# Turning batch 0's tokens with VectorE's 32x32 blocks and DMAs instead of TensorE

## What is computed

```python
y = h * sigmoid(conv(h)) @ w_out                       # h = relu(x @ w_in); 2 x 768 x 512
xn = (y - mean) / sqrt(var + 1e-6) * g_ln              # over the 512 features
out = y + relu(xn @ w_ch1) @ w_ch2                     # 512 -> 2048 -> 512
```

## Time and profile before

| | us |
|---|---|
| median of 3 runs | 467.7 |
| lowest, highest | 467.66, 473.04 |
| the profiled execution | 469.79 |
| its span | 468.1 |

### The profile page before, as it was taken

One profiled execution on the slowest core, in us unless ns is written; L12 is line 12 of the kernel. 1 busy time (PEld: TensorE's weight loads), 2 busy tenths in 40 slices (PEclk: granted clock), 3 DMA queues, 4 the chain that ended last, 5 costly groups with the idle time before them and its releaser, 6 DMA issues.

```text
span 468.1 us, 8636 instructions
## 1 busy us (share of the span) xinstructions
PE 454.7 (97%) x3119; PEld 401.5 (86%) x3119; DVE 279.7 (60%) x631; ACT 199.3 (43%) x499; POOL 269.5 (58%) x409
## 2 busy tenths in 40 slices
PE   7899889999999999999999999999999999999997
PEld 6677668999898988989889889989998999899985
DVE  4879875787676887894675543466662334243333
ACT  2988978534325756435432154224310331233110
POOL 3645788999975000077988886870024588878100
PEclk9999999999999999999999999999999999999999
DMA  9988772121201100001124432220020202220003
GB/s 226 185 200 180 185 194 60 46 86 50 91 0 46 46 1 0 1 0 45 47 91 124 124 64 95 90 81 11 1 112 22 83 10 91 90 86 6 1 0 134
DMA packets 74501, 35.17 MB, mean 75 GB/s; under 512 B 57408, under 2 KB 68700, under 8 KB 74460
## 3 DMA queue, kind: packets, MB, share of 16 engines
q1 hardware_dynamic: 70588, 33.66, 26.2%
q10 hardware_dynamic: 3872, 0.97, 0.9%
HBM read 28.72 MB, written 3.15 MB: 68 GB/s over the span
## 4 chain that ended last, share of the span: by engine, by line
PE 85%; DVE 5%; SPq 3%; issue 3%; ACT 1%; ACTq 1%; DMA 1%; POOL 0%; DVEq 0%; POOLq 0%
PE two L1493 9%; PE two L1494 9%; PE two L1492 9%; PE two L1469 8%; PE two L1472 8%; PE two L1471 8%; PE two L1319 5%; PE two L1321 5%; PE two L1320 5%; PE two L1401 5%; PE two L1400 5%; PE two L1399 5%; DVE sm L670 2%; SPq L395 2%; PE two L1304 1%
## 5 line engine op out<-in xcount | busy, mean ns | idle before, releaser
L594 POOL TENSOR_TENSOR asum<-wst 128x256 f32<-128x256 f32 x26 | 22.8, 878 | 96.3 <-PE two L1321 50.2
L1469 PE MATMUL two<-combo,wa 128*128 128x384 f32 x224 | 75.6, 337 | 1.0 <-DVE c L933 0.9
L1472 PE MATMUL two<-combo,wa 128*128 128x384 f32 x224 | 75.4, 337 | 0.0
L1494 PE MATMUL two<-wv,h 128*128 128x512 f32 x192 | 75.3, 392 | 0.0
L1493 PE MATMUL two<-wv,h 128*128 128x512 f32 x192 | 75.2, 392 | 0.0
L1471 PE MATMUL two<-combo,wa 128*128 128x384 f32 x224 | 75.2, 336 | 0.0
L1492 PE MATMUL two<-wv,h 128*128 128x512 f32 x192 | 74.7, 389 | 0.0
L1125 ACT ACTIVATE h<-u 128x384 fp32r<-128x384 f32 x32 | 16.8, 525 | 74.4 <-DVE u L915 67.5
L557 POOL TENSOR_SCALAR pn<-ex,rinv 128x120 f32<-128x120 f32 x96 | 33.5, 369 | 24.7 <-DVE rinv L683 24.7
L588 POOL TENSOR_TENSOR wa<-asum,wa 128x256 fp32r<-128x256 f32 x52 | 43.4, 836 | 4.3
L1469 PEld LDWEIGHTS two<-combo,wa 128*128 128x128 f32 x224 | 42.0, 188 | 3.2 <-issue 1.9
(11 more groups left out here) (116 smaller groups left out, 952.8 us busy)
## 6 DMA issues: line engine op xcount, KB each, us to landing
wst<-in_moe_w_ch SPq DMA_DIRECT2D x26, 512.0 KB, 3.4
vW<-in_v SPq DMA_DIRECT2D x14, 240.0 KB
kn<-in_k SPq DMA_DIRECT2D x15, 192.0 KB, 3.8
qn<-in_q SPq DMA_DIRECT2D x15, 192.0 KB, 3.7
out<-y SPq DMA_DIRECT2D x11, 256.0 KB, 2.0
wst<-in_moe_w_in SPq DMA_DIRECT2D x8, 256.0 KB, 3.4
wst<-in_moe_w_out SPq DMA_DIRECT2D x8, 256.0 KB, 2.7
tok<-xq SPq DMA_DIRECT2D x32, 48.0 KB, 2.0
```

What stands on the lines that cost most here:

```text
L1469: nc.tensor.matmul(o, wk[:, 0, kk], ck[:, 0, kk], start=(first and kk == 0), stop=False, skip_group_check=True)
L1472: ins = nc.tensor.matmul(o, wk[:, 1, kk], ck[:, 0, kk], start=False, stop=(kk == 1), skip_group_check=True)
L1494: ins = nc.tensor.matmul(o, lo, vh, start=False, stop=(f == NFP - 1 and c == 1), skip_group_check=True)
```

## The change

Batch 0 now goes batch 1's way, and both with another layout.

- `turn(b, i)` is centring and 32x32 transposition of one tile, for both batches. `xn` has three places instead of six for batch 0, so from the fourth tile on it waits for an earlier transposition.
- Its output `xq` is laid out by the destination's block row, so that each of the 16 DMAs of a half moves one run of 1536 bytes on each of 32 partitions (before: 12 runs of 128 bytes). The destination is a buffer `raw`, and ScalarE's `tokens` reads it in another order and writes `tok`.
- Batch 0: turns 0 to 2 in step 10, 3 to 5 in step 11 (VectorE); the DMAs of both halves behind load 1 on SP, the second half's also behind `hidden(12)`; all eight `tokens` in step 12 on ScalarE, four ahead of the sigmoid and four behind it. TensorE's `tokens_t` and its waits are gone.
- Batch 1: the last turn of unit 3 is moved from ahead of `c21` to behind the unit's last `h2_low`; `tokens` of the first half in unit 3 instead of 4.

```diff
-        TOK_TILE = {11: {0: 0, 1: 1, 3: 2, 4: 3}, 12: {0: 4, 1: 5, 3: 6, 4: 7}}
-        TOK_UNIT = {4: range(4), 5: range(4, 8)}
+        TOK_STEP = KF + 4
+        TOK_UNIT = {3: range(4), 5: range(4, 8)}
+        MOVED = 16 * 16
...
-        xn0 = at("xn0", [P, T, DM], F32, WIO_AT)
-        xq = at("xq", [P, KD, 3, P], F32, HG_AT + 2 * 2 * S * 4)
...
+        xn = at("xn", [P, 3, DM], F32, XT_AT + KD * HALF * 4)
+        xq = [[at("xq00", [P, 4, KD * 3, 32], F32, WIO_AT), at("xq01", [P, 4, KD * 3, 32], F32)],
+              [at("xq1", [P, 4, KD * 3, 32], F32, HG_AT + 2 * 2 * S * 4)] * 2]
+        raw = [[at("raw00", [P, 4, KD * 3, 32], F32, XT_AT + 2 * KD * HALF * 4),
+                at("raw01", [P, 4, KD * 3, 32], F32, WIO_AT + 2 * COMBO_B)],
+               [at("raw1", [P, 4, KD * 3, 32], F32, XT_AT + 2 * KD * HALF * 4)] * 2]
...
-            def move_tokens(t):
-                sp.wait_ge(xq_done, 3 * (t + 1))
-                if t == 0:
+            def move_tokens(b, t):
+                sp.wait_ge(xq_done, T * b + 3 * (t + 1))
+                if b == 0 and t == 1:
+                    sp.wait_ge(h_ready, 2 * (KF + 5))
+                elif b == 1 and t == 0:
                     sp.wait_ge(combo_done, NPROD)
+                elif b == 1:
+                    sp.wait_ge(xr_done, NSLOT + KD)
                 for a in range(4):
                     for d in range(4):
-                        src = xq[32 * a:32 * (a + 1)].rearrange("p k i (d c) -> p (k i) d c", c=32)[:, :, d]
-                        dst = tok[32 * d:32 * (d + 1), t].rearrange("p k (i a c) -> p (k i) a c", a=4, c=32)[:, :, a]
-                        sp.dma_start(dst, src).then_inc(tok_in, 16)
+                        sp.dma_start(raw[b][t][32 * d:32 * (d + 1), a].rearrange("p n c -> p (n c)"),
+                                     xq[b][t][32 * a:32 * (a + 1), d].rearrange("p n c -> p (n c)")).then_inc(raw_in[t], 16)
...
-                if l in (4, 5):
-                    move_tokens(l - 4)
+                if l == 1:
+                    move_tokens(0, 0)
+                    move_tokens(0, 1)
+                elif l in (4, 5):
+                    move_tokens(1, l - 4)
...
+            def turn(b, i):
+                n = T * b + i
                 if b == 0:
                     dve.wait_ge(h_ready, 2 * (KF + 3))
                 else:
                     dve.wait_ge(tile_proj, T * 2 * KF)
+                    dve.wait_ge(combo_done, NPROD)
+                if i >= 3:
+                    dve.wait_ge(xq_done, n - 2)
+                nc.vector.tensor_scalar(xn[:, i % 3], y[:, n], mv[:, n, 0:1], rstd[:, n:n + 1],
                                         ALU.subtract, ALU.mult).then_inc(xn_done, 1)
+                dve.wait_ge(xn_done, n + 1)
+                if b == 1 and i >= 3:
+                    dve.wait_ge(raw_in[0], MOVED * 2)
+                nc.vector.transpose(xq[b][i // 3].rearrange("p d (k i) c -> p i k d c", i=3)[:, i % 3],
+                                    xn[:, i % 3].rearrange("p (k d c) -> p k d c", k=KD, d=4)).then_inc(xq_done, 1)
...
                     if s == KF + 2:
                         inverse_std(0)
                         dve.wait_ge(rstd_done, 1)
-                        for i in range(T):
-                            centre(0, i)
+                        for i in range(3):
+                            turn(0, i)
+                    elif s == KF + 3:
+                        for i in range(3, T):
+                            turn(0, i)
                     gate(s)
...
                 elif g == 3:
-                    for i in range(3, T):
-                        centre(1, i)
-                        turn_blocks(i)
+                    turn(1, 3)
+                    turn(1, 4)
...
                 h2_low(g, 2)
                 h2_low(g, 3)
+                if g == 3:
+                    turn(1, 5)
...
-            def tokens(b, slot, src):
+            def tokens(b, slot):
                 t, k = slot // KD, slot % KD
-                if b == 0:
-                    act.wait_ge(xt_ready, slot + 1)
-                else:
-                    act.wait_ge(tok_in, 16 * 16 * (t + 1))
-                nc.scalar.activation(tok[:, t, k], src, ACT.Copy, scale=cols[:, k:k + 1]).then_inc(xr_done, 1)
+                act.wait_ge(raw_in[t], MOVED * (b + 1))
+                src = raw[b][t][:].rearrange("p a (k i) c -> p k i a c", k=KD)[:, k]
+                dst = tok[:, t, k].rearrange("p (i a c) -> p i a c", i=3, a=4)
+                nc.scalar.activation(dst, src, ACT.Copy, scale=cols[:, k:k + 1]).then_inc(xr_done, 1)
...
                 if s >= 1:
                     tap0(s)
                     if s == KF + 2:
                         root(0)
-                    for i in (0, 1, 3):
-                        if i in at_tile:
-                            tokens(0, at_tile[i], ps_h[at_tile[i] % 2][:, 0:HALF])
+                    if s == TOK_STEP:
+                        for slot in range(KD):
+                            tokens(0, slot)
                     sigmoid(s)
-                if 4 in at_tile:
-                    tokens(0, at_tile[4], ps_h[at_tile[4] % 2][:, 0:HALF])
+                    if s == TOK_STEP:
+                        for slot in range(KD, NSLOT):
+                            tokens(0, slot)
...
-                    if i in TOK_TILE.get(s, {}):
-                        pe.wait_ge(h_done, 2 * (s + 1))
-                        tokens_t(TOK_TILE[s][i], ps_h[TOK_TILE[s][i] % 2])
```

More of the change, by code:

```diff
@@ L166, in conv_gated_attention_kernel @@
         h2[1] = at("h2_1", [P, 2, 2, S], F32R, HG_AT)
-        xn0 = at("xn0", [P, T, DM], F32, WIO_AT)
-        xq = at("xq", [P, KD, 3, P], F32, HG_AT + 2 * 2 * S * 4)
-        xn1 = [at("xn1_0", [P, DM], F32, XT_AT + XT_B + SLOT_B),
-               at("xn1_1", [P, DM], F32, WIO_AT + 5 * COMBO_B)]
+        xn = at("xn", [P, 3, DM], F32, XT_AT + KD * HALF * 4)
[4 more added lines that the diff above has]
+               [at("raw1", [P, 4, KD * 3, 32], F32, XT_AT + 2 * KD * HALF * 4)] * 2]
         c21 = at("c21", [P, HALF], F32, XT_AT + 7 * HALF * 2 * 4)
         assert place[0] <= XT_AT + XT_B
-        assert HG_AT + 2 * 2 * S * 4 + 3 * DM * 4 <= EARLY_AT
+        assert HG_AT + 2 * 2 * S * 4 + 3 * DM * 4 <= EARLY_AT and 3 * DM == KD * HALF
         two = [psum2(f"two{i}") for i in range(4)]
@@ L207, in conv_gated_attention_kernel @@
         st_done, mv_done, std_done, rstd_done = sem("st_done"), sem("mv_done"), sem("std_done"), sem("rstd_done")
-        xn_done, xt_ready, xr_done = sem("xn_done"), sem("xt_ready"), sem("xr_done")
-        xq_done, tok_in = sem("xq_done"), sem("tok_in")
+        xn_done, xq_done, raw_in, xr_done = sem("xn_done"), sem("xq_done"), [sem("raw_in0"), sem("raw_in1")], sem("xr_done")
         tsum_done, ch_done, combo_done = sem("tsum_done"), sem("ch_done"), sem("combo_done")
@@ L317, in chunk_pair @@
             return l if l < NFP else l - NFP
-        def xn_home(b, i):
-            return xn0[:, i] if b == 0 else xn1[i % 2][:]
         def token_block(kh, t):
@@ L805, in inverse_std @@
                 nc.vector.reciprocal(rstd[:, r], std[:, r]).then_inc(rstd_done, 1)
-            def centre(b, i):
+            def turn(b, i):
+                n = T * b + i
                 if b == 0:
@@ L885, in _ @@
                     for i in range(3):
-                        centre(1, i)
-                        turn_blocks(i)
+                        turn(1, i)
                 dve.wait_ge(p1_done, g + 1)
@@ L1130, in _ @@
                     relu(s, 1)
-                at_tile = TOK_TILE.get(s, {})
                 if s >= 1:
@@ L1178, in _ @@
                 for slot in slots:
-                    tokens(1, slot, tok[:, slot // KD, slot % KD])
+                    tokens(1, slot)
                 for l in range(1, NLOAD):
@@ L1403, in project @@
                     ins.then_inc(tile_proj, 1)
[L1405 to L1417, removed]
             for s in range(2, 2 * KF):
@@ L1422, in _ @@
                     pe.wait_ge(x_done, NG)
-                if s - 1 in TOK_TILE:
-                    pe.wait_ge(xr_done, max(TOK_TILE[s - 1].values()))
                 pe.wait_ge(w_done, w_ready("in", s % KF))
                 hidden(s, range(KD))
-                if s - 1 in TOK_TILE:
-                    pe.wait_ge(xr_done, max(TOK_TILE[s - 1].values()) + 1)
                 hidden(s, range(KD, 2 * KD))
```

## The result

The changed kernel takes 483.2 us in the median of four runs (481.45 to 485.56), the kernel before beside it 469.5 (four runs, 467.66 to 473.04): a ratio of 1.030, 95% interval 1.025 to 1.034. It is slower by about 14 us; forecast was 469.0, with 475.0 as the upper end of the range. The profiled executions have spans of 481.9 and 468.1 us.

The account below looks back on a forecast made before the run. The prediction took TensorE, busy 97% of the span, as the bound, with VectorE close behind. Its terms, -2.94 + 2.15 + 3.0 - 0.9 = +1.3 us, gave 469.0 us, range 464.4 to 475.0.

Parts of the forecast that it names:

- A: Steps 11 and 12: TensorE's transposes of batch 0 go, a gain of 2.94 us.
- B: Step 14: batch 0's tokens come later, so TensorE waits 2.15 us before hidden(14).
- C: Unit 0: VectorE no longer keeps up, so product(0, 2) waits for p1, a loss of 3.0 us.
- D: Unit 3 of batch 1: the moved turn brings c21 earlier, less a small ScalarE delay; -0.9 us.
- The second: Rival: an issue stays at 0.665 us, lengthening the waits in step 14 and unit 3; +9.1 us, 476.8, chance 0.15.
- the 2%: Whole kernel: slower by more than two per cent, 9.4 us, needs the long issue and a little more; chance 0.04.
- The first: Rival: tokens land by 181 and VectorE loses its lag before unit 0; -4.0 us, 463.7, chance 0.25.
- the third: Rival: batch 0's new pattern takes VectorE 1.4 us a transposition; +6.5 us, 474.2, chance 0.08.

Follow-up runs that it names:

- probe_issue: The kernel before with 34 extra DMAs on SP's queue in steps 9 to 15, in eight groups differing in shape and source; 470.1 us in one run.
- eight_dmas: The changed kernel with 8 DMAs of 64 partitions a half instead of 16 of 32, tokens permuted; 471.2 us, ratio 1.005.
- unit4: The changed kernel with the tokens of batch 1's first half in unit 4 again; 477.95 us, ratio 1.020.
- eight_combo: eight_dmas with two of the three combo_low of step 14 moved behind gate(15); 467.0 us, ratio 0.996.
- before_turn: The kernel before with only batch 1's last turn moved behind the last h2_low of unit 3; 467.3 us, ratio 0.9963; run again, 467.6 us, 0.9983.
- pool_sums: unit4 with 8 of batch 0's 16 DMAs a half on GpSimd, and a token sum and combos moved behind gate(15) or p1; 470.4 us, ratio 1.006.

## Why the prediction was wrong

- **A, right.** Forecast 2.94 us, measured 2.95. The turns' price was right too: batch 0's transposition in four dimensions takes 0.71 us, and VectorE was done with the sixth at 174.24, 11.6 us after its first turn began; the sum had 11.7.
- **B, right mechanism, wrong size; this is the step that failed.** The sum took p = 0.40 us for an issue, "nearest to the rows with long runs". It measured 0.663. The rows of 0.33 and 0.37 were DMAs with one end in memory, the 0.62 the only one of my rows between SBUF and SBUF; I took the length of the runs for what made the difference, and so the low end. `probe_issue` shows that the length has hardly a part in it (median issue 0.59 us with one run of 1536 bytes, 0.61 with six of 128), and `eight_dmas` that the number of issues sets the stall. At 0.665 the text had 6.1 us for B, and 8.8 were measured: my second half began when it was ready, at 175.35, but at that price SP issues the first half until 167.3 + 16 x 0.665 = 177.9, and the second half queues up behind it. By the forecast's own times the last issue is then at 167.3 + 31 x 0.665 = 187.9 instead of 185.3, which is the missing 2.6 us. So two things failed in this step: the price of an issue, and the queueing of the second half behind the first.
- **C, right mechanism; its size hung on B.** Forecast 3.0 us, 1.8 measured in the changed kernel, 0.3 in `unit4` with the same code up to there, 3.7 where step 14's stall is gone (`eight_dmas`), and 2.5 of these are VectorE's queue (`eight_combo`). That 3.0 lies between them is in part luck.
- **D, wrong sign by the same p.** Forecast -0.9 us, at 0.665 +2.9; measured +3.92, with 0.626 us an issue here and the slow stretch that the forecast didn't have. The last token landed at 272.47, 11.4 us after the first issue. The moved turn by itself gives what the text gave it (`before_turn`, `unit4`).
- **What no step had: the clock.** After each of the three waits TensorE ran for a stretch at 1.2 GHz, which cost 1.37 us in step 14, 1.6 in unit 0, and about 1.7 within unit 3's 3.92. That is 4.7 us of the 13.9. The forecast took a stall at its own length.
- **The rivals.** The second, the issue no shorter, is what happened. It had +9.1 us and a chance of 0.15; the queueing and the clock were missing in it too, and with them it lies beyond the 2% that the text gave 0.04. The first (the service engines keep up) and the third (the new pattern is dear) didn't happen.

## What to carry to other kernels

Price a DMA's issue by rows with the same two ends, not by the nearest size: here an SBUF to SBUF copy cost its queue 0.6 us whatever it carried, so 16 copies are 10 us of queue; what shortened the wait in these runs was fewer copies or a second queue. Work taken off the busiest engine is won only as far as the engines that take it over have slack at that place; look at what is queued behind each wait that they get, and at the next step's need. Where the busiest engine must stand for microseconds, add to the wait what its clock can lose behind it: here up to 2.35 us (step 14 of `unit4`, 10.66 instead of 8.31).

## What the runs showed of the hardware

- The issue of a DMA between SBUF and SBUF takes SP 0.48 to 0.65 us in `probe_issue`, for 4 to 96 KB, 16 to 128 partitions and runs from 128 to 1536 bytes; from memory to 32 partitions 0.35 to 0.42. In the kernels that use such copies the median is 0.59 to 0.62 us, and single issues took up to 1.5. GpSimd issues the same copy in 0.52 us with its gap. The median from issue to landing of a group was 1.7 to 2.5 us.
- TensorE's granted clock fell to 1.2 GHz for a stretch, during or behind single waits of 1.8, 3.3, 3.6, 3.7, 5.3 and (twice) 8.8 us. In the gated part and the third stage it stayed at 2.4 GHz through waits of 0.5, 0.7, 0.89 and 1.2 us, but also, in `pool_sums`, through one of 1.18 us and one of 2.57 us that ended 6 us apart. In `probe_issue` it fell at about 59 us, in the attention stage, where no wait between 50 and 64 us was longer than 0.98 us. So the length of a wait alone doesn't tell whether the clock falls; what does stays open here. In the changed kernel the low clock cost 16 to 87% of the wait itself (1.37 us after 8.8, 1.6 after 1.8).
- A 32x32 block transposition of 128x512 values takes VectorE 0.71 us in the old layout (three dimensions) and in the new one (four).
